# The start of an attention kernel: first keys and their tails stacked before the queries, and three high parts made by VectorE

## The reference, cut to what matters

```python
q_rot, k_rot = (rotate(q), rotate(k))        # x1*cos - x2*sin, x1*sin + x2*cos
scores = np.matmul(q_rot, k_rot.transpose(0, 1, 3, 2)) / np.sqrt(D)
attn = np.exp(scores - np.max(scores, axis=-1, keepdims=True))
attn = attn / (np.sum(attn, axis=-1, keepdims=True) + 1e-09)
out = np.matmul(attn, v)
```

## Time and profile before

| what | value |
|---|---|
| time, median of 3 runs | 921.51 us (921.14 to 922.54) |
| the profiled execution | 921.68 us, span 919.9 us |
| TensorE busy | 909.6 us, 99% of the span |
| VectorE busy | 696.2 us, 76% |
| GpSimd busy | 558.2 us, 61% |
| ScalarE busy | 543.8 us, 59% |
| first score of the first pair starts | 14.22 us |
| granted TensorE clock | 1.00 throughout |

### The profile page before, as it was taken

One profiled execution on the slowest core, in us unless ns is written; L12 is line 12 of the kernel. 1 busy time (PEld: TensorE's weight loads), 2 busy tenths in 40 slices (PEclk: granted clock), 3 DMA queues, 4 the chain that ended last, 5 costly groups with the idle time before them and its releaser, 6 DMA issues.

```text
span 919.9 us, 18291 instructions
## 1 busy us (share of the span) xinstructions
PE 909.6 (99%) x6201; PEld 843.3 (92%) x6201; DVE 696.2 (76%) x1151; ACT 543.8 (59%) x1186; POOL 558.2 (61%) x550
## 2 busy tenths in 40 slices
PE   8999999999999999999999999999999999999998
PEld 6999999999999899998898899899888989989897
DVE  5898898988999899832777788789998572663624
ACT  4999999999998565634555655565564222212111
POOL 5999998999967467565656578758976210010100
DMA  6343343343231333000000000001300001010011
GB/s 182 84 110 85 83 109 83 76 113 85 74 105 49 105 104 92 24 2 1 1 1 1 1 1 1 1 24 50 114 0 2 1 1 46 1 51 9 1 46 58
DMA packets 48982, 45.52 MB, mean 49 GB/s; under 512 B 17996, under 2 KB 38988, under 8 KB 48780
## 3 DMA queue, kind: packets, MB, share of 16 engines
q1 hardware_dynamic: 48540, 44.10, 17.3%
q10 hardware_dynamic: 368, 0.46, 0.2%
HBM read 28.81 MB, written 4.72 MB: 36 GB/s over the span
## 4 chain that ended last, share of the span: by engine, by line
PE 89%; DVE 6%; ACT 1%; issue 1%; POOL 1%; DMA 1%; SPq 1%; POOLq 0%; ACTq 0%
PE fc_ps L2261 16%; PE seven_ps L2291 15%; PE ring_ps L2132 9%; PE scores_ps L2068 7%; PE wide_ps L2460 6%; PE ring_ps L2079 6%; PE bank_ps L2416 6%; PE wide_ps L2439 6%; PE bank_ps L2478 5%; PE seven_ps L2341 2%; DVE lefts L1734 2%; PE seven_ps L2261 2%; DVE hid_sums L1722 2%; PE ring_ps L2013 2%; PE scores_ps L2061 2%; DVE winS L1866 1%
## 5 line engine op out<-in xcount | busy, mean ns | idle before, releaser
L2261 PE MATMUL fc_ps<-xT,W1s 128*128 128x512 f32 (+1 forms) x828 | 191.0, 379 | 0.4 <-ACT hid L1240 0.3
L2291 PE MATMUL seven_ps<-rights,lefts 128*128 128x256 f32 x1344 | 173.6, 284 | 0.0
L2291 PEld LDWEIGHTS seven_ps<-rights,lefts 128*128 128x128 f32 x1344 | 169.5, 191 | 4.4
L2261 PEld LDWEIGHTS fc_ps<-xT,W1s 128*128 128x128 f32 x828 | 146.2, 189 | 27.7 <-ACT hid L1240 1.3
L1547 DVE TENSOR_REDUCE nmax<-scores_ps 128x1 f32<-128x576 f32 x144 | 106.8, 752 | 16.9 <-PE scores_ps L2068 13.7
L1025 POOL TENSOR_TENSOR rights<-w_rest,rights 128x256 fp32r<-128x256 f32 x84 | 80.9, 963 | 54.2 <-ACT rights L1283 54.2
L1132 ACT ACTIVATE E<-scores_ps,nmax 128x576 f32<-128x576 f32 x128 | 95.6, 748 | 8.5 <-DVE nmax L1547 7.7
L1087 POOL TENSOR_TENSOR rstd<-ve,power 128x1 f32<-128x1 f32 x18 | 14.4, 798 | 138.9 <-DVE ve L1916 138.9
L1556 DVE TENSOR_TENSOR prob_lo<-ring_ps,prob_hi 128x512 fp32r<-128x512 f32 x144 | 95.4, 682 | 3.8 <-ACT prob_hi L1146 2.5
L2068 PE MATMUL scores_ps<-stack 128*128 128x288 f32 x384 | 87.7, 315 | 1.0 <-DMA swapped_k<-stack 0.7
L1146 ACT ACTIVATE prob_hi<-ring_ps 128x512 fp32r<-128x512 f32 x144 | 85.3, 611 | 1.3 <-PE ring_ps L2079 0.5
(11 more groups left out here) (197 smaller groups left out, 2080.2 us busy)
## 6 DMA issues: line engine op xcount, KB each, us to landing
stack<-stack SPq DMA_DIRECT2D x32, 144.0 KB, 2.5
w_raw<-in_w SPq DMA_DIRECT2D x18, 256.0 KB, 2.9
swapped_k<-stack SPq DMA_DIRECT2D x31, 144.0 KB, 2.4
qk_raw<-in_k SPq DMA_DIRECT2D x16, 256.0 KB
qk_raw<-in_q SPq DMA_DIRECT2D x16, 256.0 KB
v_raw<-in_v SPq DMA_DIRECT2D x16, 256.0 KB, 2.8
w_rest<-in_w SPq DMA_DIRECT2D x7, 512.0 KB, 4.1
out<-out_sb SPq DMA_DIRECT2D x14, 256.0 KB, 2.4
```

The costliest lines, as they stand in the source:

```text
L2261: mm = nc.tensor.matmul(fc1_bank(n, f)[:, 0:cols], W1s[:, slot1(f), w, c, :], xT[:, x, c, 0:cols], start=first, stop=(c == DC - 1 and x == 1))
L2291: mm = nc.tensor.matmul(seven_ps[k][:, 2 * P * a:2 * P * (a + 1)], lefts[:, k, x, P * a:P * (a + 1)], rights[:, k, w, :], start=(g == 0 an ...
```

## The change

Four things change, all of them for the first two pairs only.

1. TensorE transposes the tail of the first keys right behind the first keys (round -1), and that of the queries where both stood before. ScalarE copies the two keys' tails by themselves (`first_keys`, before the high part of the first queries), the queries' tails later. Both halves of the first swap are issued by SyncE, after the keys' tails.
2. In `first_rope` the low part of the keys moves ahead of the query products, and the sum of the other head's keys ahead of the low part of the queries.
3. The high parts of the second pair and of the first values become VectorE's: keys after the fifth maximum of round 0, queries and values after the sixth.
4. TensorE's fillers: 14 instead of 17 at the start, 9 instead of 2 at the end of round -1.

```diff
@@ SyncE: swap_keys(p, h)
-                wait_freed(sp, p, *latest(stack_order, ("TL", 0), ("K", h)))
-                swap_main(sp, p, h, (1,) if is_round(p, 0) and h == 0 else (0, 1))
+                if is_round(p, 0) and h == 0:
+                    wait_freed(sp, p, "K", 0)
+                    sp.wait_ge(first_key_tails_kept, 1)
+                else:
+                    wait_freed(sp, p, *latest(stack_order, ("TL", 0), ("K", h)))
+                swap_main(sp, p, h)
@@ ScalarE
-                tails = stack[:, p.odd, 0:4 * TAIL_STEP].rearrange("p (n t) -> p n t", n=4)[:, :, 0:TAIL]
-                read_out(nc.scalar.activation(tails, bank("TL", 0)[:, 0:4 * TAIL].rearrange("p (n t) -> p n t", n=4), ACT.Copy), "TL", 0)
+                read_out(copy_tails(p, slice(0, 2 if is_round(p, 0) else 4)), "TL", 0)
+
+            def copy_tails(p, which):
+
+                tails = stack[:, p.odd, 0:4 * TAIL_STEP].rearrange("p (n t) -> p n t", n=4)[:, which, 0:TAIL]
+                return nc.scalar.activation(tails, bank("TL", 0)[:, 0:4 * TAIL].rearrange("p (n t) -> p n t", n=4)[:, which], ACT.Copy)
...
             def v_high(p):
-                if not live(p):
+                if not live(p) or is_round(p, 0):
                     return
...
-            def second_high(r, which):
-                if not is_round(r, 0):
-                    return
-                act.wait_ge(rope_step, count(rope_order, r + 1, ("add", which), 1))
-                wait_filled(act, r, ("QK"[which], 0), ("QK"[which], 1), ("TL", 0))
-                nc.scalar.activation(qk_split[:, which, :, 0:D], rot[:, which], ACT.Copy).then_inc(split_hi[which], 1)
...
             first_high(1)
-            first_high(0)
+
+            def first_keys(p):
+
+                if not is_round(p, 0):
+                    return
+                act.wait_ge(zeroed_rows, 1)
+                act.wait_ge(first_key_tails, 1)
+                copy_tails(p, slice(2, 4)).then_inc(first_key_tails_kept, 1)
+                first_high(0)

             def body(r):
...
                 copy_stack(r, 0, 1)
+                first_keys(r)
                 copy_stack_tails(r)
-                if is_round(r, 0):
-                    wait_freed(act, r, *latest(stack_order, ("TL", 0), ("K", 0)))
-                    swap_main(act, r, 0, (0,))
@@ VectorE: first_rope
                 first_add(1, own)
+                dve.wait_ge(first_hi, 1)
+                first_low(0, 1, own)
                 dve.wait_ge(qk_in[0][0], 48)
                 first_products(0, own)
                 dve.wait_ge(first_rot, 7)
                 first_add(0, own)
-                dve.wait_ge(first_hi, 1)
-                first_low(0, 1, own)
                 first_products(1, other)
+                dve.wait_ge(first_rot, 11)
+                first_add(1, other)
                 dve.wait_ge(first_hi, 2)
                 first_low(0, 0, own)
-                dve.wait_ge(first_rot, 11)
-                first_add(1, other)
                 first_products(0, other)
@@ VectorE
+            def second_high(r, which):
+
+                if not is_round(r, 0):
+                    return
+                dve.wait_ge(rope_step, count(rope_order, r + 1, ("add", which), 1))
+                wait_filled(dve, r, ("QK"[which], 0), ("QK"[which], 1), ("TL", 0))
+                nc.vector.tensor_copy(qk_split[:, which, :, 0:D], rot[:, which]).then_inc(split_hi[which], 1)
+
+            def first_v_high(r):
+
+                if not is_round(r, 0):
+                    return
+                dve.wait_ge(v_in, 48)
+                nc.vector.tensor_copy(v_split[:, r.odd, :, 0:D], v_raw[:, :, :]).then_inc(v_hi, 1)
...
                 maximum(r, 4)
+                second_high(r, 1)
                 denominators(r - 1)
                 reciprocals(r - 1)
                 maximum(r, 5)
+                second_high(r, 0)
+                first_v_high(r)
@@ TensorE: make_stack_tails(p)
+                if is_round(p, 0):
+
+                    pe.wait_ge(first_lo[0][0], 1)
+                    stack_tail(0).then_inc(filled, 1)
+                    return
...
+            def stack_tail(which):
+                return nc.tensor.transpose(bank("TL", 0)[:, P * which:P * which + P].bitcast(f32r),
+                                           qk_split[:, which, NT, :], ident_r[:, :])
...
-            idle(17)
+            idle(14)
...
                 if is_round(r, -1):
-                    idle(2)
+                    stack_tail(1).then_inc(first_key_tails, 1)
+                    idle(9)
```

More of the change, by code:

```diff
@@ L288, in attention_and_mlps @@
         v_hi = sem("v_hi")
+        first_key_tails = sem("first_key_tails")
+        first_key_tails_kept = sem("first_key_tails_kept")
         v_lo = sem("v_lo")
@@ L478, in wait_loaded, with swap_main @@
             eng.wait_ge(qk_in[p.odd][which], p.i * 16 + (48 - 32 * p.odd))
-        def swap_main(eng, p, h, halves=(0, 1)):
+        def swap_main(eng, p, h):
             keys = stack[:, p.odd, KEYS[h]:KEYS[h] + S]
-            for half in halves:
+            for half in range(2):
                 to, src = D * half, D * (1 - half)
@@ L1204, in body @@
                 exp(r, 2)
-                second_high(r, 1)
                 prob_high(r - 1, "G2", 1)
@@ L1210, in body @@
                 exp(r, 3)
-                second_high(r, 0)
                 v_high(r)
@@ L2020, in make_stack_tails @@
                     return
+                if is_round(p, 0):
+                    pe.wait_ge(first_lo[0][0], 1)
+                    stack_tail(0).then_inc(filled, 1)
+                    return
                 for which in range(2):
[L2022 to L2025, removed]
+                    pe.wait_ge(split_lo[which], p.i)
                 wait_freed(pe, p, "TL", 0, before=1)
                 for which in range(2):
-                    mm = nc.tensor.transpose(bank("TL", 0)[:, P * which:P * which + P].bitcast(f32r),
-                                             qk_split[:, which, NT, :], ident_r[:, :])
+                    mm = stack_tail(which)
                 mm.then_inc(filled, 1)
+            def stack_tail(which):
+                return nc.tensor.transpose(bank("TL", 0)[:, P * which:P * which + P].bitcast(f32r),
+                                           qk_split[:, which, NT, :], ident_r[:, :])
             def stacked_keys(p, h, at, size):
```

## The result

| | before | changed kernel |
|---|---|---|
| median (lowest to highest, runs) | 922.54 us (921.14 to 923.46, 9) | 926.08 us (924.05 to 928.88, 9) |
| the profiled execution, its span | 921.68 us, 919.9 us | 928.88 us, 927.1 us |
| granted clock in it | 1.00 | 0.996 |
| first score | 14.22 us | 18.41 us |

The ratio is 1.0046, with a 95% interval of [1.0038, 1.0055]: slower, by 3.5 us between the medians, where 921.4 was forecast.

The account below looks back on a forecast made before the run. TensorE, 99% busy, gains only before its pipeline fills, with GpSimd and ScalarE within a microsecond. The first score's 0.3 us gain is spent by 24 us; 0.1 remains: 921.6 for the profiled execution, forecast 921.4, range 920.4 to 922.8.

Parts of the forecast that it names:

- GpSimd starts no earlier: At the start, GpSimd gets in only at VectorE's wait; its chain moves by +0.2 us, rotary sums at 19.8 and 21.2.
- one sum less to do behind it: VectorE's start sequence: query low part ends 0.57 us later, but one sum less (0.34) follows, so 0.23 later.
- Cost nothing: GpSimd late by 1.7 us after pair 1; pair 2's queries end at 41.05, taken at 42.10, so no cost.
- The tails of pair 1: TensorE's tails of pair 1 follow GpSimd's query low part at 25.45 us; before they ran at 25.48.
- the row at 38.21: VectorE's 9-element scalar operation, 1.17 us against a median of 0.154, ending with GpSimd's low part; used to price waiting casts.
- GpSimd's lag outlives its slack: Rival: both second-part delays make GpSimd some 3 us late, 2 beyond slack less idle: about 922.5 to 923; chance 0.05.
- the first rival: VectorE's moved casts aren't held by GpSimd; tails and seventh maximum come 1.0 us earlier: 920.5; chance 0.16.
- The casts: High parts moved to VectorE: 0.46 us for 576 elements, plus the whole rest of whichever GpSimd product is running.
- The transfer: First key swap: 3.1 us from issue to first score, so keys there at 12.9 and first score at 13.9.
- ScalarE's relief: ScalarE loses three copies and a wait, 2.25 us, but waits for pair 1's tails, leaving 0.1 us gained.

Follow-up runs that it names:

- experiment 6: GpSimd's release moved in the changed kernel (925.97 and 925.14 us) and the kernel before (922.63); in the kernel before, sum put ahead of query low part (926.20).
- experiment 2: Changed kernel with GpSimd released by VectorE's last low part of the first pair (924.13 us), or with the sum back behind the query low part (924.87 us).
- second part: Kernel before with only the high parts of pair 1 and of the first values moved to VectorE: 924.72 us, ratio 1.0030.
- experiments 3 and 5: 3: row sums by reduction in the second part (922.46 us) and the kernel before (921.91). 5: changed kernel repaired, without reduction 922.52, with it 921.06.
- all repairs: Changed kernel with GpSimd released late, pair 1's query loads behind the first swap, and row sums by reduction: 921.06 us, ratio 0.9985.
- experiment 5: Changed kernel with GpSimd released late and query loads behind the swap: 922.52 us; with the reduction too 921.06; without it, high parts back on ScalarE, 922.66.
- first part: Changed kernel with the three high parts back on ScalarE: 923.87 us, ratio 1.0020.
- fillers: Changed kernel with fifteen more TensorE fillers ahead of the second head's keys: 926.06 us, ratio 1.0039.
- both moved releases: Changed kernel with GpSimd released by the first low part of the keys (925.97 us), or by the thirteenth step of VectorE's first rotary (925.14 us).
- exchange: Kernel before with only the other key head's sum put ahead of the first query low part: 926.20 us, ratio 1.0047.
- its reduction: The second part alone with the row sums made by a one-element reduction instead of a scalar operation: 922.46 us, ratio 1.0005.
- before's reduction: Kernel before with the row sums made by a one-element reduction instead of a scalar operation: 921.91 us, ratio 0.9997.
- sum back: Changed kernel with the sum of the other head's keys back behind the first query low part: 924.87 us, ratio 1.0034.
- release at 13: Kernel before with GpSimd's rotary of pair 1 released by the thirteenth product of VectorE's first rotary: 922.63 us, ratio 1.0003.
- later release: Changed kernel with GpSimd's first products waiting for VectorE's last low part of the first pair: 924.13 us, ratio 1.0023.

## Why the prediction was wrong

**The step that failed is "GpSimd starts no earlier".** I took the 3.29 us product for the rule that GpSimd gets in only at VectorE's first wait, and priced the new order at +0.2 us. The rule held only for the old order. With the sum ahead of the query low part GpSimd got in at once, and it was VectorE that waited: first score +4.19 instead of -0.3. Exchanging these two instructions gives this in the kernel before (experiment 6), exchanging them back removes it (experiment 2; the 14.87 there is the transfer). I had noticed "one sum less to do behind it", but counted its 0.34 us as work and didn't ask what its place did to the competition. No rival held this case. What was missing is one in which GpSimd gets in at once, and each of the seven instructions that VectorE still had takes about one GpSimd product.

**The second failure is "Cost nothing" in the second part.** The tails of pair 1 were right: 25.45 forecast, 25.35 in the second part alone. GpSimd's lag there was 1.55 us at pair 2 (1.7 forecast). I let the queries of pair 2 absorb it, and they did (ready at 40.90, taken at 43.59); but I had used the row at 38.21 only as a price for the casts, without asking when it comes again. It stands in the path of round 1, GpSimd's lag lengthens it, and TensorE waits for what exceeds about 1.4 us. The reduction took that cost away (experiments 3 and 5). How much of the second part's 2.6 us it is stays open: its one profile shows 0.31 us of it, the medians with the reduction 2.3. "GpSimd's lag outlives its slack" had the right cause at 0.05, with the wrong place.

**The casts** of 576 elements neither waited for GpSimd's products, as forecast, nor took 0.46 us, as the first rival had it: they took 0.74, the first with GpSimd idle, the second (22.67) in the middle of its low part. I had drawn a line through 0.284 us for 256 elements and 0.428 for 512; the nearest row for what they took was a maximum over 576 elements, 0.76. The cast of the values did wait for the running product, as forecast: with all repairs it lasts 0.99 us, ending 0.35 after GpSimd's first low part (23.21), and GpSimd's second, begun at 23.18, shows 1.65 us instead of 1.4. GpSimd's low parts behind the first cast came 1.3 us later than before (22.23 against 20.92). The Trainium skill (VectorE: DVE Perf Modes, section "Mode 2×_2P — use both read ports for one tensor") says that the two-port mode needs outermost dimensions that are even, or odd and equal on both sides. The 576 elements are nine tiles, dense in the source and strided among the low parts in the destination; the 256 are four tiles. The measured 0.74 and 0.28 agree, but no run changed the shape alone.

**The transfer** was mis-sized: 4.1 to 4.9 us under the loads in the changed kernel against 3.1 taken from before. With the loads behind it, it took 2.4, and then the queue of TensorE decided, as forecast: 13.59, where I had 13.9.

**ScalarE's relief** of 2.25 us was held to be worth 0.1. Without the reduction the runs agree (922.52 against 922.66, experiment 5); with it, relief and reduction together are worth 1.6 us.

**What stays open.** The sum stood ahead of the low part, with GpSimd released near 10 to 11 us, in six profiles, and GpSimd got in at once in all six (changed, first part, fillers, both moved releases, exchange); it stood behind in six, and GpSimd was held in all six (before, second part, its reduction, before's reduction, sum back, release at 13). Why this order matters is not shown: in both groups it arrived 0.05 to 0.26 us ahead of VectorE's next row, and with the release at 13 it arrived 0.26 and 0.25 us into the same cross products, and got in once and was held once. Nor is it shown why the values' cast got its turn between two GpSimd low parts, where the scalar operation on the row sums waited for both.

## What to carry to other kernels

A long first duration on GpSimd beside a busy VectorE is one outcome of two, not a rule: before reordering VectorE's instructions near a GpSimd release, price both outcomes, and where the loss is large, fix the order by a wait. An engine's lag isn't free when its consumer has slack; look for every short operation on another engine that its busy time holds up, and check whether a form that isn't held exists. A transfer moved earlier may move into the loads and take twice as long: order the queue's issues with it.

## What the runs showed of the hardware

- With GpSimd in, VectorE's two-input instructions of 0.4 us go at one for each GpSimd product (0.9 to 1.7 us each), and its casts of 0.28 take 0.87 to 1.53, while GpSimd's own products lengthen only from about 1.42 to between 1.45 and 1.61.
- The scalar operation on nine elements waited for the whole unbroken chain of GpSimd instructions, not for the running one: it ended within 0.05 us of the chain's end at 39.38, 40.94, 41.66, 42.99 and 45.95. TensorE waited only for what exceeded about 1.4 us of it. The Trainium skill (SBUF — State Buffer, section "Who interferes with whom") names the exclusion; that it can last over several instructions is seen here (2.90 us over two). A reduction of the same nine elements took 0.14 us in such a chain.
- The two transfers of 144 KB of the first swap took 2.4 us each with the loads issued behind them and 4.1 to 5.4 us with the loads ahead. In the order of before they took 2.6 to 3.1 us when issued at 11.10, up to 3.5 when issued at 10.6 (second part), and up to 4.5 when issued at 10.2 and 10.4 (second part and kernel before, with the reduction).
- After TensorE's idle 3.75 us the granted clock of the changed kernel read 0.50 from about 15 to 21.6 us and 1.00 later; in the first part alone, after the same idle time, from about 16 to 19.4. In the two kernels with the reduction and the start of before it read 0.50 from 16 to 19 us after 2.1 us idle. Waits of 1.50, 1.75 and 1.93 us at the same place (later release, sum back, release at 13) left it at 1.00.
